# A repeated pair of work units in the second layer, written out twice or run as a loop on three engines

## The reference

```python
for t in range(S):                                 # B=2, H=8, S=768, D=64
    state = gamma[None, :, None, None] * state + np.einsum('bhd,bhe->bhde', k[:, :, t], v[:, :, t])
    y[:, :, t] = scale * np.einsum('bhd,bhde->bhe', q[:, :, t], state)
...
P = np.exp(logits)                                 # first mixture: N=1536, D=512, E=8, F=1024
for _ in range(8):
    P /= P.sum(1, keepdims=True) + 1e-09
    P /= P.sum(0, keepdims=True) + 1e-09
    P *= N / E
for e in range(E):
    out += P[:, e:e + 1] * (np.maximum(x @ w1[e], 0.0) @ w2[e])
...
p = domain_probs / (domain_probs.sum(-1, keepdims=True) + 1e-09)   # second mixture: E=4
for e in range(E):
    out += p[:, e:e + 1] * (np.maximum(x @ w1[e], 0.0) @ w2[e])
```

## Time and profile before

| | |
|---|---|
| median of 3 runs | 1502.83 us (1502.57 to 1503.82) |
| the profiled execution's own time | 1502.83 us |
| its span, first to last instruction | 1501.1 us |
| PE busy | 1492.6 us, 99% |
| PEld, DVE, ACT, POOL busy | 1452.5, 1063.2, 759.1, 310.7 us |
| TensorE's granted clock over the span | 1.0 |
| instruction records | 26117 |

### The profile page before, as it was taken

One profiled execution on the slowest core, in us unless ns is written; L12 is line 12 of the kernel. 1 busy time (PEld: TensorE's weight loads), 2 busy tenths in 40 slices (PEclk: granted clock), 3 DMA queues, 4 the chain that ended last, 5 costly groups with the idle time before them and its releaser, 6 DMA issues.

```text
span 1501.1 us, 26117 instructions
## 1 busy us (share of the span) xinstructions
PE 1492.6 (99%) x10250; PEld 1452.5 (97%) x10250; DVE 1063.2 (71%) x1401; ACT 759.1 (51%) x1297; POOL 310.7 (21%) x261
## 2 busy tenths in 40 slices
PE   9999999999999999999999999999999999999999
PEld 8999989999999999999999999999999999999998
DVE  7756856668767786787687777676478768777763
ACT  5422323556556555565565565343355556556531
POOL 6100001322232123122221221012112322132100
PEclk9999999999999999999999999999999999999999
DMA  9100101343343334333433343301023443334321
GB/s 354 60 28 30 57 1 57 92 92 99 71 96 86 98 77 95 80 98 86 96 73 95 91 91 94 76 3 55 29 72 98 92 92 83 87 92 92 99 64 64
DMA packets 44848, 123.48 MB, mean 82 GB/s; under 512 B 3168, under 2 KB 3680, under 8 KB 44768
## 3 DMA queue, kind: packets, MB, share of 16 engines
q0 software_dynamic: 10368, 56.63, 19.1%
q1 hardware_dynamic: 34256, 65.65, 12.3%
q10 hardware_dynamic: 144, 0.10, 0.0%
HBM read 62.59 MB, written 3.15 MB: 44 GB/s over the span
## 4 chain that ended last, share of the span: by engine, by line
PE 93%; issue 3%; POOL 2%; DMA 1%; DVE 1%; ACT 0%; SPq 0%; POOLq 0%; DVEq 0%
PE psum L1894 12%; PE psum L1892 12%; PE psum L1890 12%; PE psum L1862 11%; PE psum L1864 11%; PE psum L1866 11%; PE psum L1805 4%; PE psum L1806 4%; PE psum L1804 4%; PE psum L1780 4%; PE psum L1784 4%; PE psum L1782 4%; POOL q_up L569 1%; DMA w_raw<-in_moe_w 0%; DVE w_lo L1127 0%
## 5 line engine op out<-in xcount | busy, mean ns | idle before, releaser
L1894 PE MATMUL psum<-w_hi,h_lo 128*128 128x256 f32 x1512 | 427.8, 283 | 0.0
L1892 PE MATMUL psum<-w_lo,h_hi 128*128 128x256 f32 x1512 | 427.7, 283 | 0.0
L1890 PE MATMUL psum<-w_hi,h_hi 128*128 128x256 f32 x1512 | 427.6, 283 | 0.0
L1862 PE MATMUL psum<-x_hi,w_hi 128*128 128x384 f32 x1008 | 337.1, 334 | 2.6 <-DVE h_raw L1356 2.6
L1864 PE MATMUL psum<-x_lo,w_hi 128*128 128x384 f32 x1008 | 336.8, 334 | 0.0
L1866 PE MATMUL psum<-x_hi,w_lo 128*128 128x384 f32 x1008 | 336.8, 334 | 0.0
L1894 PEld LDWEIGHTS psum<-w_hi,h_lo 128*128 128x128 f32 x1512 | 290.0, 192 | 0.0
L1892 PEld LDWEIGHTS psum<-w_lo,h_hi 128*128 128x128 f32 x1512 | 289.9, 192 | 0.0
L1890 PEld LDWEIGHTS psum<-w_hi,h_hi 128*128 128x128 f32 x1512 | 289.8, 192 | 0.0
L1127 DVE TENSOR_TENSOR w_lo<-w_raw,w_hi 128x512 fp32r<-128x512 f32 (+1 forms) x131 | 125.9, 964 | 124.4 <-ACT w_hi L934 123.6
L1862 PEld LDWEIGHTS psum<-x_hi,w_hi 128*128 128x128 f32 x1008 | 189.4, 188 | 3.5 <-issue 3.4
(11 more groups left out here) (157 smaller groups left out, 2430.7 us busy)
## 6 DMA issues: line engine op xcount, KB each, us to landing
acc<-staged POOLq DMA_DIRECT2D x72, 768.0 KB, 5.7
w_raw<-in_moe_w SPq DMA_DIRECT2D x46, 1024.0 KB, 5.1
kt_in<-in_k_t SPq DMA_DIRECT2D x12, 256.0 KB, 6.9
qt_in<-in_q_t SPq DMA_DIRECT2D x12, 256.0 KB, 8.5
v_in<-in_v SPq DMA_DIRECT2D x12, 256.0 KB, 8.7
k_in<-in_k SPq DMA_DIRECT2D x10, 256.0 KB, 9.0
out<-acc SPq DMA_DIRECT2D x2, 768.0 KB, 3.6
out<-acc SPq DMA_DIRECT2D x5, 256.0 KB, 2.0
```

Of the source, the lines that this page charges most:

```text
L1862: nc.tensor.matmul(o, w1_hi[:, w, kc, fs], x_hi[:, x, kc, at], start=start and kc == 0, stop=False, skip_group_check=True)
L1890: nc.tensor.matmul(o, h_hi[:, h, kc, rows], w2_hi[:, v, kc, :], start=product in (D_P1, D_P4) and kc == 0, stop=False, skip_group_check=True)
L1892: nc.tensor.matmul(o, h_hi[:, h, kc, rows], w2_lo[:, v, kc, :], start=False, stop=False, skip_group_check=True)
L1894: last = nc.tensor.matmul(o, h_lo[:, h, kc, rows], w2_hi[:, v, kc, :], start=False, stop=kc == 1, skip_group_check=True)
```

## The change

The two pairs of fast units in the second mixture become a hardware loop of two rounds on ScalarE, VectorE and TensorE. SyncE and GpSimd are not touched.

```diff
@@ ScalarE @@
             fast_unit(FAST_2, N_FAST_1, gate2, 0)
-            for i in range(E2 - 2):
+            with act.Fori(0, E2 - 2) as i:
                 fast_unit(2 * i + (FAST_2 + 1), 2 * i + (N_FAST_1 + 1), gate2, i + 1)
                 fast_unit(2 * i + (FAST_2 + 2), 2 * i + (N_FAST_1 + 2), gate2, i + 1)
             fast_unit(L2_LAST - 1, N_FAST - 1, gate2, E2 - 1)
@@ VectorE @@
-            for i in range(E2 - 2):
+            with dve.Fori(0, E2 - 2) as i:
@@ TensorE @@
-            for i in range(E2 - 2):
+            with pe.Fori(0, E2 - 2) as i:
                 fast_unit(2 * i + (FAST_2 + 1), 2 * i + (N_FAST_1 + 1))
                 fast_unit(2 * i + (FAST_2 + 2), 2 * i + (N_FAST_1 + 2))
```

## The result

| | before | changed |
|---|---|---|
| median | 1503.07 us (5 runs) | 1512.10 us (5 runs) |
| ratio | | 1.0058, 95% interval 1.0047 to 1.007 |
| span of the profiled execution | 1501.1 us | 1510.2 us |
| PE busy | 1492.6 us | 1494.4 us |

The change makes the kernel 9.0 us slower. I had forecast no change (1502.8, range to 1505.0). What happened is the first rival, to which I gave 0.07. Of all the runs in this document one was slow (one of E7's four, 1830.05 us at a mean granted clock of 0.75, against 0.99 to 1.00 in the others, for which I have no explanation); its median and ratio leave it out.

What follows compares the result with a forecast made beforehand. PE's matmul issue was taken to bound the kernel; body, entry, back edge, exit and fetches summed to 0.00 us, so 1502.83 + 0 gave 1502.8 us, range 1501.8 to 1505.0.

Steps and rivals of the forecast that it cites:

- the first rival: TensorE's back edge misses its code because the head's packet was overwritten; 1505.8 us, chance 0.07.
- What bounds the kernel: Whole kernel: PE is busy 1492.6 of 1501.1 us, so time is the number of matmuls by their pace.
- Register operations, entry, exit, fetch traffic at zero: New loop: computed waits, loop entry and exit, and about 7 fewer q8 packets each cost 0 us.
- The back edge at zero: New loop's one back edge costs 0 on PE, ACT and DVE, as read from four in the first loop.
- The place of the new head: New loop on TensorE: head 36 instructions earlier within its packet than the first loop's, at -2 to 13, most likely inside.
- The price of a miss: TensorE's back edge: one fetch of 5.1 us less 2.1 in hand, 3.0 us, bounds 0 to 7.5.
- The cover of 2.1 us: At the back edge, TensorE's sequencer has 2.1 us of queued matmuls in hand.
- The two-page rule: The skill's rule that taken branches outside a two-page window force a fetch: a single stall here, given 0.02.
- ACT or DVE late: ACT's or DVE's back edge misses its code, costing 4.1 us, bounds 0.7 to 8.6; 1506.9 us, chance 0.03.

Runs made afterwards that it cites:

- E7: The changed kernel with the head of TensorE's new loop put at slot 239 of its 256-instruction code packet by branched-over padding; 1513.92 us, ratio 1.0073.
- E2: The changed kernel with only ScalarE and VectorE running the new loop, TensorE's pairs written out; 1503.28 us, ratio 1.0.
- E3: The changed kernel with the head of TensorE's new loop put at slot 0 of a code packet by branched-over padding; 1503.12 us, ratio 0.9998.
- E8: The kernel before the change, with the head of the first mixture's loop on TensorE moved to slot 128; 1533.37 us, ratio 1.0204.
- E6: The changed kernel with TensorE's new loop head at slot 128, so the body ends 79 instructions into an eighth packet; 1510.58 us, one run.
- E5: The changed kernel with TensorE's new loop head at slot 52, so the body ends 3 instructions into an eighth packet; 1502.46 us, one run.
- E10: The changed kernel with 4 more instructions on TensorE ahead of its new loop; 1502.72 us, ratio 0.9996.
- E1: The changed kernel with only TensorE running the new loop, ScalarE's and VectorE's pairs written out; 1511.78 us, ratio 1.0058.
- E11: The changed kernel with TensorE's new loop head at slot 80, so the body ends 31 instructions into an eighth packet; 1509.7 us, one run.

## Why the prediction was wrong

*What bounds the kernel* held: TensorE's issue, and whatever interrupts it, adds up one for one.

*Register operations, entry, exit, fetch traffic at zero* held: round one is 118.69 us, E2 and E3 are level with the kernel before.

*The back edge at zero* is the term that failed: 8.7 us where I had 0. Four equal back edges in the trace were one measurement of one position, not four of a rule, and E8 shows the same loop paying at each of them.

*The place of the new head* is the step behind it that is at fault. The distance between the heads, 36 slots short of whole packets, was right. The place of the first one, estimated from the times of code packets at 34 to 49 slots in, was not: with the new head at 252, it is 32. From there its body of 1743 instructions ends 17 short of an eighth packet, so the first loop itself runs free by little. By the slots now known, a packet was seen starting 0.2 us after its predecessor was entered in E6 (1251.8 and 1252.0) and 3.8 us after in the changed kernel (1244.4 and 1248.2); at 0.06 us an instruction that is a spread of 60 instructions, too much to give a slot. The estimate of -2 to 13 had its lower end outside the packet, the head stands at -4, just below it, and I still gave the miss 0.07. The mechanism of the first rival was the right one: a head at the very end of a packet, a body that touches one packet more than in the first loop, and the head's packet overwritten.

*The price of a miss* was mis-sized: 3.0 us in the rival's sum (bounds 0 to 7.5), 8.7 measured. The fetch was priced by a weight load (5.1 us), and the branch takes 6.3. Left out were the second packet's stall (2.5 to 2.8 us), which comes because the head's packet held only 4 instructions of the loop, and the slow clock after standing still (1.2). The cover of 2.1 us held: in E6, with one stall, the hole is 4.58 us, and 6.3 - 2.1 is 4.2, near it.

*The two-page rule* that the prediction weighed is still not what the runs show: E3, E5 and E10 branch back over seven packets in 0.22 us. It stands in the Trainium skill ("Runtime: NRT & Kernel Launch", section "Instruction fetch mechanics"). The section's other figure, 2048 instructions for TensorE in blocks of 256, fits all twelve experiments, and so does its warning that a taken branch to code not at hand stalls; here the branch takes 6.3 to 6.7 us.

*ACT or DVE late* was wrong as a cause, by E1 and E2. Whether their loops could miss at other positions was not tried.

## What to carry to other kernels

A loop body of 1743 instructions on TensorE, which is always busy here, is free or costs 6 to 10 us per back edge, by where its first instruction falls among the 256-instruction code packets; any edit ahead of it moves that. If a body comes near eight packets, fix the head's slot or halve the body, and read the compare-and-branch's duration in the profile: 0.2 us is a hit, 6.3 to 6.7 a miss. When you fix the slot, leave more than a few instructions between the head and its packet's end, or the entry stalls too (E7, with 17). A neighbour loop that runs free is evidence for its own position only.

## What the runs showed that I had not expected

- A miss is not one stall but a whole round of refetching (9 packets in round two of the changed kernel, 36 over E8's four back edges, none in E3). It is hidden except at the head, and again at the next packet where few instructions lie between: 2.5 us of idle weight loads behind 1 load, 0.8 behind 7.
- Holes of 4.4 to 7.4 us each brought TensorE back at 0.32 us a matmul for 9 matmuls (the changed kernel) and 18 (E6), 1.2 to 2.8 us more. The single stall has the longer slow stretch, because in both the granted clock fell while TensorE still stood idle, and in the changed kernel the second stall used up over half of the low stretch. Stretches of the changed kernel, then of E6; the clock is the number behind the last bracket:

```profile
1258.73:1261.90 3.17, 0.00 (x0) 0.00 (x0) 1.21 (x1) 0.75 (x2) 3.01 (x3) 1.00 0.65 127
1261.90:1266.08 4.18, 0.00 (x1) 0.29 (x1) 0.00 (x0) 0.00 (x0) 1.37 (x2) 0.50 0.39 78
1266.08:1268.72 2.64, 2.64 (x9) 2.64 (x9) 0.00 (x0) 0.48 (x1) 0.00 (x0) 0.50 0.94 186
```

```profile
1258.77:1262.24 3.47, 0.00 (x1) 0.00 (x0) 1.21 (x1) 0.75 (x2) 3.31 (x3) 1.00 0.60 118
1263.19:1269.07 5.88, 5.88 (x18) 5.88 (x19) 0.00 (x0) 1.07 (x3) 0.86 (x1) 0.50 0.70 137
```

  In E11 the clock is back already at 1266.7, after one stall and 11 matmuls; why so early is open.
- The body may run 3 instructions into the eighth packet unharmed (E5) but not 31 (E11).
